# Attention scores moved to SBUF by the row-maximum pass, whole-row exponentials, and the expert gate folded into each head's output

## The reference

```python
q, k, v: (2, 8, 1152, 64)            # 16 heads in all; float32
q_pool = q.reshape(B, H, S // 2, 2, D).mean(axis=3)        # 576 queries a head
scores = (1 / 8) * q_pool @ k.T                            # 576 x 1152
attn = exp(scores - scores.max(-1)); attn /= attn.sum(-1) + 1e-9
x = (attn @ v) -> (1152 tokens, 512)                       # 8 heads side by side
# layer 1: N=1152, D=512, E=8, F=1024, capacity 288
logits = x @ w_gate; expert = argmax; gate = softmax(logits)[expert]
tokens go to their expert in order until it is full; y = relu(xe @ w1[e]) @ w2[e]
x = gate * y (0 for dropped tokens)
# layer 2: P = exp(x @ w_gate2 - max), eight rounds of row and column normalisation
out = sum over e of P[:, e] * (relu(x @ w1[e]) @ w2[e])
```

## Time and profile before

| what | us |
|---|---|
| time, median of 3 runs (lowest, highest) | 1431.06 (1431.04, 1433.53) |
| the profiled execution: span from its first to its last instruction | 1427.8 |
| what lies between that span and the median of the runs | 3.3 |
| busy in the span: PE / PEld / DVE / ACT / POOL | 1369.6 / 1255.5 / 539.9 / 568.7 / 442.0 |
| heads | about 11 to 340 |
| last head's end to the first expert's matmuls | 341 to 376 |
| first layer's experts, hand-over, second layer's experts | 376 to 1428 |

### The profile page before, as it was taken

How to read it: one execution, slowest core, us unless ns; L and a number is a source line. 1 busy time by engine, 2 the same in 40 slices (tenths; PEclk the granted TensorE clock), 3 DMA queues, 4 the chain that set the end, 5 groups by cost and what they waited for, 6 DMA issues and landing times.

```text
span 1427.8 us, 23661 instructions
## 1 busy us (share of the span) xinstructions
PE 1369.6 (96%) x8156; PEld 1255.5 (88%) x8156; DVE 539.9 (38%) x1215; ACT 568.7 (40%) x1433; POOL 442.0 (31%) x422
## 2 busy tenths in 40 slices
PE   7999999999599999889999999999999999999999
PEld 5888888888599999879899999999999999999998
DVE  6888888886222222142631212122222221212121
ACT  6888888886345554421221221311311312212211
POOL 5322332221967775730230220310501402202200
PEclk9999999999699999989999999999999999999999
DMA  3711111100765665430020110110200300200001
GB/s 94 224 51 51 41 34 50 50 30 8 253 193 158 210 204 181 153 124 1 30 89 0 60 59 0 59 59 0 88 29 1 116 0 31 87 0 0 0 0 66
DMA packets 66413, 103.00 MB, mean 72 GB/s; under 512 B 3888, under 2 KB 22900, under 8 KB 66361
## 3 DMA queue, kind: packets, MB, share of 16 engines
q1 hardware_dynamic: 58424, 86.03, 18.7%
q10 hardware_dynamic: 6464, 11.80, 2.5%
q0 software_dynamic: 1472, 4.54, 1.0%
HBM read 88.38 MB, written 14.16 MB: 72 GB/s over the span
## 4 chain that ended last, share of the span: by engine, by line
PE 88%; ACT 4%; issue 3%; DVE 3%; DMA 1%; ACTq 0%; DVEq 0%; SPq 0%; POOL 0%; POOLq 0%
PE psum L1320 34%; PE psum L1333 28%; PE psum L1352 7%; PE psum L1110 5%; PE psum L1136 5%; PE psum L1121 4%; ACT small L544 1%; ACT acts L520 1%; PE psum L1146 1%; DVE mx L760 1%; PE psum L1365 1%; PE psum L1088 1%; PE psum L1209 1%; PE psum L1310 1%; DVE acts L751 0%
## 5 line engine op out<-in xcount | busy, mean ns | idle before, releaser
L1320 PE MATMUL psum<-acts,wsplit 128*128 128x384 f32 (+1 forms) x3072 | 515.4, 326 | 2.5 <-issue 1.5
L1320 PEld LDWEIGHTS psum<-acts,wsplit 128*128 128x128 f32 x3072 | 505.7, 189 | 5.0 <-issue 1.8
L1333 PE MATMUL psum<-wsplit,acts 128*128 128x512 f32 x1728 | 397.7, 390 | 0.0
L1333 PEld LDWEIGHTS psum<-wsplit,acts 128*128 128x128 f32 x1728 | 323.7, 188 | 66.3
L654 ACT ACTIVATE acts<-psum 128x384 fp32r<-128x384 f32 (+1 forms) x256 | 120.7, 471 | 569.1 <-PE psum L1320 563.8
L443 POOL TENSOR_TENSOR wsplit<-raw,wsplit 128x512 fp32r<-128x512 f32 x128 | 162.5, 1293 | 535.4 <-ACT wsplit L520 535.4
L931 DVE SCALAR_TENSOR_TENSOR acts<-psum,acts 128x384 fp32r<-128x384 f32 (+1 forms) x256 | 136.1, 532 | 373.5 <-ACT acts L654 369.1
L448 POOL TENSOR_TENSOR wsplit<-raw,wsplit 128x512 fp32r<-128x512 f32 x128 | 161.0, 1295 | 133.6 <-ACT wsplit L520 133.6
L520 ACT ACTIVATE wsplit<-raw 128x512 fp32r<-128x512 f32 (+1 forms) x257 | 154.8, 625 | 86.6 <-PE psum L1333 75.2
L520 ACT ACTIVATE acts<-psum 128x384 fp32r<-128x384 f32 (+2 forms) x282 | 131.2, 465 | 68.4 <-PE psum L1310 22.4
L1063 DVE SCALAR_TENSOR_TENSOR x<-psum,pr,x 128x512 f32<-128x512 f32 x63 | 47.4, 752 | 293.5 <-PE psum L1333 293.5
(11 more groups left out here) (128 smaller groups left out, 606.9 us busy)
## 6 DMA issues: line engine op xcount, KB each, us to landing
raw<-in_moe_w_dram SPq DMA_DIRECT2D x64, 1024.0 KB, 5.1
raw<-in_k_dram SPq DMA_DIRECT2D x16, 288.0 KB, 2.8
raw<-in_v_dram SPq DMA_DIRECT2D x16, 288.0 KB, 3.8
slots_in<-zero SPq DMA_DIRECT2D x1, 4608.0 KB
small<-slots_in ACTq DMA_DIRECT2D x8, 576.0 KB, 4.7
small<-in_q_dram SPq DMA_DIRECT2D x16, 256.0 KB, 3.0
slots_out<-small ACTq DMA_DIRECT2D x7, 576.0 KB, 6.9
out_dram<-x ACTq DMA_DIRECT2D x9, 256.0 KB, 2.4
```

What stands on the lines that cost most here:

```text
L1320: last = mm(psum[:, f % HBANKS, 0:w], w1s[a][:, c, f * P:(f + 1) * P], src[z][:, c, cols], start=(i == 0), stop=(i == 3 * DC - 1))
L1333: last = mm(psum[:, bank, :], hs[a][:, f, t0:t0 + P], w2s[z][:, f, :], start=(i == 0), stop=(i == 3 * FC - 1))
```

## The change

What it does, part by part:

- **Row maximum and move.** `row_max` becomes `move_scores`: a `tensor_scalar` that multiplies by 1.0, writes the chunk from PSUM to `prob` in SBUF, and gives the running minimum through its accumulator output (the queries are scaled with a negative sign, so the minimum is the maximum); the first chunk has no second operand, the next two take the minimum so far as pointer operand. The small joining reduce goes.
- **Exponential.** One `activation` of 1152 columns per query tile, in place in `prob`, with scale -1.0 and one row sum. `prob` has four buffers, two of them in `raw`, where w1 lay.
- **Banks and order.** Three banks for scores, freed by the move, and three for transposes. TensorE's order per tile: nine transposes of tile t, six score matmuls of tile t + 2, then `prep` or `turn_out`, then `values`. The other engines' lists follow; `prep` stands a tile earlier.
- **Gate in the turn of the output.** `gfold` holds per head the fold matrix (64 columns) and the gate's rows of that head (8 columns), so `turn_out` gives outputs and that head's share of the logits; `finish` writes both, `choose` first adds eight shares. Token transposes, copies and gate matmuls are gone.
- **Routing and loads.** Batch 0 is chosen in tile 0 and placed in tile 2 of the last head, its scatter follows at once; w1 of the first expert is loaded after the last transposes of probabilities.

```diff
-    QSCALE = float(DH) ** -0.5 / 2
+    QSCALE = -(float(DH) ** -0.5) / 2
+        FD = DH + E
+        gfold = rawf[:, GF0:GF0 + G * FD].rearrange("p (g c) -> p g c", g=G)
-        prob = [small[:, 4 * QP + i * S:4 * QP + (i + 1) * S] for i in (0, 1)]
+        rawl = raw[:, 0:2, :].rearrange("p a w -> p (a w)")
+        NP = 4
+        prob = [small[:, 4 * QP + i * S:4 * QP + (i + 1) * S] for i in (0, 1)] + \
+               [rawl[:, i * S:(i + 1) * S] for i in (0, 1)]
-        BPT, BPV, BMISC = 4, 6, 7
+        BPT, TBANKS, BPV, BMISC = 3, 3, 6, 7
-        SBANKS, HBANKS = 4, 4
+        SBANKS, HBANKS = 3, 4
...
             load_w2(0, 0, 0)
+            sp.wait_ge(pt_ready, SCH * G)
+            load_w1(0, 0, 0)
+            load_w1(0, 0, 1)
...
+            pool.tensor_copy(gfold[:, :, 0:DH], fold[:, :].unsqueeze(1).broadcast_to([P, G, DH])).then_inc(fold_ready, 1)
...
-            for f in range(FC // 4):
-                lo_w1(0, f)
-
             pool.wait_ge(zeroed, 32)
+            scatter_rows(0)
+            for f in range(FC // 4):
+                lo_w1(0, f)
+            scatter_rows(1)
...
+            def exps(g, v, t):
+                u, b = v % 2, buf(v, t)
+                act.wait_ge(s_moved, SCH * g + NC * (t + 1))
+                if t == 0 and not (isinstance(g, int) and g < 2):
+                    act.wait_ge(den_step, DS * (g - 2) + 1)
+                nc.scalar.activation(prob[b], prob[b], ACT.Exp, bias=low[:, b, NC - 1:NC], scale=-1.0,
+                                     accum_out=sums[:, u, t:t + 1]).then_inc(exp_done, 1)
...
             def head(g, v):                                             # ScalarE
                 for t in range(QT):
+                    if t == 0 and not first:
+                        evac_ot(g - 1, 0)
+                    if t == 2 and not first:
+                        evac_ot(g - 1, 1)
                     for c in range(NC):
+                        p_hi(g, v, t, c)
+                    if not (last and t == QT - 1):
+                        exps(*ahead(g, v, t, 1))
+                    if t < PREP - 1 and not last:
+                        prep_evac(g + 1, 1 - v % 2, t + 1)
+                    if t == QT - 1 and not (last or isinstance(g, int) and g == G - 2):
+                        prep_evac(g + 2, v % 2, 0)
...
+            def move_scores(g, v, t, c):
+                b = buf(v, t)
+                if c == 0 and not (is_first(g) and t < NP):
+                    dve.wait_ge(pt_ready, SCH * g + NC * (t - NP + 1))
+                if c:
+                    dve.wait_ge(s_moved, SCH * g + NC * t + c)
                 dve.wait_ge(s_ready, SCH * g + NC * t + c + 1)
+                nc.vector.tensor_scalar(prob[b][:, c * CH:(c + 1) * CH], psum[:, chunk(v, t, c) % SBANKS, 0:CH],
+                                        1.0, low[:, b, c - 1:c] if c else None, ALU.mult, ALU.min,
+                                        accum_out=low[:, b, c:c + 1]).then_inc(s_moved, 1)
...
             def head(g, v):                                             # VectorE
                 for t in range(QT):
                     for c in range(NC):
+                        p_lo(g, v, t, c)
+                        if not (last and t >= QT - 2):
+                            move_scores(*ahead(g, v, t, 2), c)
+                        if t == 0 and not first:
                             row_sums(g - 1, 1 - v % 2, c)
+                    if t < PREP - 1 and not last:
+                        prep_evac(g + 1, 1 - v % 2, t + 1)
+                    if t == 0 and last:
+                        choose(0)
+                    if t == 2 and last:
+                        place(0)
+                    if t == 3 and not first:
                         finish(g - 1)
...
             def scores(g, v, t, c):
+                if t in (0, 3) and c == 0:
+                    pe.wait_ge(misc_free, misc_prep(g, PREP - 2 if t == 0 else PREP - 1) + 1)
                 if not (is_first(g) and m < SBANKS):
-                    pe.wait_ge(exp_done, SCH * g + NC * t + c - SBANKS + 1)
+                    pe.wait_ge(s_moved, SCH * g + NC * t + c - SBANKS + 1)
             def turn_probs(g, v, t, c):
+                pe.wait_ge(exp_done, QT * g + t + 1)
+                if not (is_first(g) and m < TBANKS):
+                    pe.wait_ge(pl_done, SCH * g + NC * t + c - TBANKS + 1)
...
+            BESIDE = {0: (None, (0, 8)), 1: ((8, 13), (13, VSTEPS)),
+                      2: (None, (0, 5)), 3: ((5, 8), (8, 11)), 4: ((11, 14), (14, VSTEPS))}
+            def misc(g, v, t):
+                if t < PREP - 1:
+                    if not is_last(g):
+                        prep(g + 1, 1 - v % 2, t + 1)
+                    elif t == 1:
+                        pe.wait_ge(misc_free, misc_out(G - 3) + 1)
+                        prefix(0)
+                elif t == PREP - 1:
+                    if is_last(g):
+                        pe.wait_ge(idx_done, 2)
+                    if not is_first(g):
+                        turn_out(g - 1)
+                elif not (is_last(g) or isinstance(g, int) and g == G - 2):
+                    prep(g + 2, v % 2, 0)
...
             def head(g, v):                                             # TensorE
                 for t in range(QT):
+                    nxt = not (last and t >= QT - 2)
+                    for c in range(NC):
+                        turn_probs(g, v, t, c)
+                    for c in range(NC):
+                        if nxt:
+                            scores(*ahead(g, v, t, 2), c)
+                    misc(g, v, t)
                     beside(g, v, t, 0)
                     beside(g, v, t, 1)
```

More of the change, by code:

```diff
@@ L248, in misc_after_prep, with ahead, buf @@
         def misc_after_prep(h):
[L249 to L255, removed]
+            return misc_prep(h, PREP - 1) + 1
+        def ahead(g, v, t, n):
+            return (g, v, t + n) if t + n < QT else (g + 1, (v + 1) % 4, t + n - QT)
+        def buf(v, t):
+            return (QT * v + t) % NP
         def gcol(t):
@@ L470, in _, with scatter_rows @@
             split_values(G - 1, 1)
-            for f in range(FC // 4):
-                lo_w1(0, f)
-            pool.wait_ge(zeroed, 32)
-            for b in range(B):
+            def scatter_rows(b):
                 pool.wait_ge(idx_done, 2 * b + 1)
-                pool.wait_ge(den_step, 4 * (G - 2) if b < B - 1 else 4 * G)
+                pool.wait_ge(den_step, DS * NH * (b + 1))
                 for t in range(QT):
@@ L806, in head @@
                     for c in range(NC):
-                        if not (first and t == 0):
-                            p_lo(*before(g, v, t), c)
-                        if not (last and t == QT - 1):
-                            row_max(*after(g, v, t), c)
-                        if t == QT - 1 and not first:
-                            row_sums(g - 1, 1 - v % 2, c)
-                    if t < PREP and not last:
-                        prep_evac(g + 1, 1 - v % 2, t)
-                    if t < EARLY and last:
-                        dve.wait_ge(early_ready, t + 1)
-                        dve.wait_ge(lg_tail, 1)
-                        nc.vector.tensor_copy(lg[:, t, :], psum[:, BMISC, 0:E]).then_inc(early_done, 1)
@@ new lines, in beside @@
+            def beside(g, v, t, part):
+                if BESIDE[t][part] is None:
+                    return
+                if t >= 2:
+                    values(g, v, 0, *BESIDE[t][part])
+                elif not is_first(g):
+                    values(g - 1, (v - 1) % 4, 1, *BESIDE[t][part])
+            def misc(g, v, t):
[12 more added lines that the diff above has]
+                    prep(g + 2, v % 2, 0)
@@ L1229, in head @@
             def head(g, v):
[L1230 removed]
+                last = is_last(g)
                 for t in range(QT):
[L1232 to L1236 removed]
+                    nxt = not (last and t >= QT - 2)
+                    for c in range(NC):
+                        turn_probs(g, v, t, c)
+                    for c in range(NC):
+                        if nxt:
+                            scores(*ahead(g, v, t, 2), c)
+                    misc(g, v, t)
                     beside(g, v, t, 0)
[L1238 to L1241 removed]
                     beside(g, v, t, 1)
[L1243 to L1248 removed]
             pe.wait_ge(consts, 16)
```

297 lines of the change are left out of this document (68 added, 229 removed).

## The result

Median 1389.82 us (4 runs, 1389.54 to 1390.22) against 1431.05 (4 runs, 1430.94 to 1433.53): ratio **0.9708**, 95% interval 0.9694 to 0.9722. The profiled span is 1387.9 against 1427.8, 39.9 less; forecast were 37.9 less and 1393 us.

The account below looks back on a forecast made before the run. No engine full; the loop through four score banks, held from matmul to exponential, sets the pace. Heads -26.6, last head -3.2, hand-over -8.1: span 1427.8 to 1389.9, plus 3.3 gives 1393 us, own range 1385 to 1402.

Parts of the forecast that it names:

- TensorE is the bound once the waits go: Attention heads: 18.0 us of TensorE work in 20.50 a head, about 2.5 of stalls; 18.6 a head after the change.
- Rival B: Heads: TensorE was the bound all along, only 1.2 us a head of named stalls go; 1403 us, chance 0.08.
- A: Heads: VectorE becomes the bound, a move costing 0.72 to 0.80, 19.2 to 20.2 us a head; 1403 to 1417, chance 0.20.
- m: VectorE's cost in us of one 384-column move with row maximum: 0.62 taken, bounds 0.46 and 0.80, passing TensorE's pace at 0.68.
- rival C: Heads: better than forecast, moves at 0.50 and no collisions, 17.9 to 18.2 us a head; 1385 or 1382, chance 0.14.
- Ring and collisions, +0.6 a head: Heads: transposes, p_hi, exponential take 3.07 and bind tile 2 alone (+0.2); collisions on VectorE's queue add 0.4.
- Exponential, start to the end of the read 1.37: ScalarE in the heads: one 1152-column exponential takes 1.37 us from its start to the end of its accumulator read.
- Last head 17.3 (-3.2): Last attention head: 17.3 us against 20.5, token transposes and gate matmuls gone; less gain if TensorE waits for the place step.
- Hand-over 23.0: From last value block to first transposes of expert rows: 23.0 us against 31.15, a gain of 8.1.
- Clock: Low granted clock when work restarts at 370 to 380 us: cost left as it is, 3 us to either side.
- heads 1 to 14: Fourteen full attention heads at 18.6 us, 1.90 less than now each: -26.6 us.
- Rival D: Heads: slower, VectorE's list of 7.95 + 15m outweighs the gains from a move of 0.89; 1457 us at 1.0, chance 0.05.

Follow-up runs that it names:

- Run 9: Changed kernel with one extra small reduce on VectorE behind each move: 1406.32 us, ratio 0.9817.
- run 6: Changed kernel with the exponential as three of 384 columns per tile instead of one of 1152: 1390.99 us, ratio 0.9704.
- run 1: Changed kernel with batch 0's token count and place step moved later, so TensorE waits for neither: 1386.43 us, ratio 0.9678.
- Runs 1, 2 and 3: The third is the changed kernel with both edits, batch 0's place step later and VectorE's heads written out without loop: 1384.34 us, ratio 0.9665.
- run 11: Changed kernel with late place step, VectorE's heads written out, and GpSimd's w1 low halves held until choose(1) has ended: 1383.45 us, ratio 0.9652.
- run 10: Changed kernel with two extra small reduces on VectorE behind each move: 1482.11 us, ratio 1.0342.
- run 2: Changed kernel with VectorE's list of sixteen heads written out, no hardware loop: 1386.67 us, ratio 0.9679.

## Why the prediction was right, point by point

The 39.9 us of the span, cut where the rows allow it: up to the finish of head 1 -6.4 (64.81 against 71.22; some 3 of it only because `finish` now stands a tile earlier in the head), twelve regular distances -31.1, the loop's stands +3.2, the last distance -0.9 (19.58 against 20.50), from there to the last value block +1.7, the hand-over -8.45, behind it +2.0.

- **TensorE is the bound once the waits go: right.** 18.0 of work was forecast, 17.91 is what a head takes. Rival B had the same bound at a wider distance, and falls; A falls with the size of m. Run 9 shows VectorE's list 2.5 us away, run 6 that more work on ScalarE costs nothing. No run takes work off TensorE; that it is the bound rests on these two and on its blocks standing end to end.
- **m = 0.62: mis-sized, 0.51.** The read was priced by ScalarE's 0.09; it costs the engine nothing that shows. The lower bound had been 0.46, plus 0.04 for the pointer: nearly that. It did not move the time, since m decides only from 0.68. This was one half of rival C, the likeliest of whose numbers, 17.9 to 18.2 a head, hold. VectorE: DVE Perf Modes of the Trainium skill (section "Two Vector instructions with no wait between them") calls such an operation two instructions, and the trace agrees. The rule of the same page of the Trainium skill (section "The DRAIN you can't avoid"), by which the next operation waits for an empty pipe, isn't borne out between these neighbours (0.55 long, followed after 0.47); that section itself excepts operations that are not held, which the prediction's "every" left out.
- **Ring and collisions, +0.6 a head: the ring right, the collisions nothing.** The ring transposes, p_hi, exponential takes 3.16 from 166.77 (forecast 3.07): the read of tile 2's exponential ends at 169.93, and the next transposes start at 169.98. So tile 2 can't be shorter, though a stand of 0.23 inside it is all that the waits list. No collision is left of the 0.4, likely because with a move at 0.51 the p_lo behind it comes 0.3 a tile earlier. And the work of 18.0 was 0.4 too much: nine transposes cost 0.94 to 1.02 where 1.17 was priced, the output 1.17 for 1.25, six scores 0.98 to 1.01 where 0.87 was. That 17.91 lies at 18.0 is in part luck: it is 17.6 of work and 0.3 of ring. That no collisions came is the other half of C. Taken together, 18.6 against 17.91 is 9.7 us over 14 heads (14 x 0.69), the largest error of the sum.
- **Exponential, start to the end of the read 1.37: right,** 1.35 (165.99 - 164.64). Run 6 adds that its gain of ScalarE time buys nothing, and that SBUF in place of PSUM costs 0.05, inside the 0.1 of the forecast.
- **Last head 17.3 (-3.2): wrong, 19.58 by the finish steps.** From its first transposes to the last value block it took 22.10 before, 22.25 in the changed kernel and 17.32 in run 1. The step that failed is the one left as a condition: "If TensorE has to wait for the place step before the output, this shrinks by 1 to 2." It does wait, 2.06, and then loses about 3 more at 1.2 GHz up to the last value block, of which the condition had nothing; a lower clock inside the head stood in no term of the sum. Run 1 gives 16.52 from finish to finish without either, 0.8 under the forecast.
- **Hand-over 23.0: right, 22.70.** Term by term, with the forecast in brackets: value block to finish 5.48 (5.76), new reduce 0.80 (0.4), reduce to indices 3.84 (4.15), wake-up of GpSimd 0.79 (1.1), five scatters 5.15 (4.9: a slot is 1.28 from start to start, not 1.22), to the expert rows 6.64 (6.63). The first expert doesn't wait for w1: the waits of 330 to 380 us have no such row.
- **Clock: inside its 3 us.** Work behind the restart takes 2.0 more than before, with one more short stretch at the lower level near 621 us (0.64 in 620 to 624). Runs 1, 2 and 3 have it as well, run 11 hasn't. TensorE shows as busy in all of 600 to 640 us there, so no wait that shows brings this one. What decides on it stays open.
- **Not in the forecast:** the stands at the loop, 3.2 us. The kernel before had two such stands on ScalarE, 3.2 us together, and the distances of its finish steps stay at 20.2 to 20.8 over them: ScalarE's slack covered them.

Since `finish` has moved, the parts are set against the forecast by the first transposes of a head, which have not (head 1: 32.99 before, 31.91 now; head 15: 319.15 and 285.54). Scores now run one tile further ahead of them, so between the first row and the fourth about 1 us may stand in the wrong one:

| part | forecast | measured |
|---|---|---|
| head 0 | 0 | -1.1 |
| heads 1 to 14, without the stands | -26.6 | -35.7 |
| stands at the loop | none | +3.2 |
| last head | -3.2 | +0.1 |
| hand-over | -8.1 | -8.4 |
| behind the restart | 0 | +2.0 |
| sum | -37.9 | -39.9 |

The parts were further off than the sum, whose span came out 2.0 lower: that 1393 lies so near 1390 is in part luck, a gain of 10 us more than forecast in the heads against 8.5 us of losses that the forecast did not have.

Rival D is a real mechanism of this kernel: run 10 has a move of 0.51 + 0.53 = 1.04, for which D's formula gives a head of 7.95 + 15 x 1.04 = 23.6; 23.35 is measured, and the whole is 3.4% slower than before. The accumulator was simply cheap.

## What to carry to other kernels

When waits of one engine are taken away, add up that engine's work from starts of blocks, and ask of every other engine how far its list lies below; that distance, not its busy share, tells what an instruction may cost. A deeper lead needs the banks on both sides of the engine: here the third transposing bank decided more than the whole gain. A wait for bookkeeping placed ahead of work at the end of a stage can be paid twice, as here: once as the wait (2.06) and again by the clock behind it (about 3).

## What the hardware showed that I had not expected

- A move with an accumulator costs VectorE 0.48 to 0.53 us for 384 columns out of PSUM, the read of 0.08 nothing on top.
- VectorE stands for 3.04 and 2.46 us where its loop over four heads goes round; written out, it doesn't (run 2). Advanced Engine Details and Errata of the Trainium skill (section "Control Flow Timing") gives a compare-and-branch about 0.1 us, so the branch alone isn't it; whether it is the fetching of instructions was not tried.
- GpSimd holds VectorE up. An 80-column tensor_tensor with both inputs in SBUF took 2.30 beside two of GpSimd's (run 1) and 0.24 without them (run 11); one of 5 columns took 0.93 beside them and 0.17 without. Both ended within about 0.1 us of GpSimd's second. A 40-column one in run 11 was through when GpSimd's first was (0.37). Beside the pair an operation that reads PSUM, and reduces, were not held: 0.20 as always. The other way about nothing shows: GpSimd's took 1.26 to 1.33 each in the changed kernel and in runs 1 and 11. SBUF — State Buffer of the Trainium skill (section "Who interferes with whom") says that a VectorE instruction with two SBUF inputs contends with a GpSimd one that reads SBUF, and that the later one is blocked in full; the trace agrees. Whether it is let in between two of GpSimd's that follow each other went either way here (2.30 and 0.37).
- A wait of 2.06 us in a stretch with TensorE 72% busy was followed by 6.5 us at 0.50 of the clock, in which the same ten loads took 2.14 instead of 1.25; with the wait gone (run 1) the stretch kept 1.00. In run 2, where the wait stays (2.06), the low stretch stays too. The stretch near 621 us shows that the lower level also comes where TensorE is shown busy throughout.
